# Tiles a quarter of a unit sooner, another order in units 0 and 1, and unread fp32 products in three waits of TensorE

## What is computed

```
for t in range(S):                       # 768 steps; B=4, H=8, D=48
    S_re, S_im = ar*S_re - ai*S_im + kv, ar*S_im + ai*S_re     # kv = k[t] outer v[t]
    y[t] = q[t] @ S_re                   # ar, ai: a_re, a_im scaled to magnitude <= 0.999
x = y as (3072, 384)
h = x @ w_in                             # (384, 2048)
g = where(h >= 1, h, where(h <= -1, 0, (h + 1)**2 / 4));   x = g @ w_out     # first layer
P = exp(x @ w_gate - max); eight times: rows normalised, columns normalised  # gate
out = sum over e of P[:, e] * (relu(x @ w1[e]) @ w2[e])                      # second layer
```

## Time and profile before

| | |
|---|---|
| median of 3 runs | 2300.43 us |
| lowest, highest | 2298.07, 2301.52 us |
| the profiled execution | 2298.59 us, its span 2296.8 us |
| mean granted TensorE clock | 0.994 of full |
| busy share of the span | PE 97%, DVE 75%, ACT 44%, POOL 20% |

### The profile page before, as it was taken

One profiled execution on the slowest core, in us unless ns is written; L12 is line 12 of the kernel. 1 busy time (PEld: TensorE's weight loads), 2 busy tenths in 40 slices (PEclk: granted clock), 3 DMA queues, 4 the chain that ended last, 5 costly groups with the idle time before them and its releaser, 6 DMA issues.

```text
span 2296.8 us, 37984 instructions
## 1 busy us (share of the span) xinstructions
PE 2226.7 (97%) x13699; PEld 2075.5 (90%) x13699; DVE 1733.0 (75%) x3049; ACT 1006.9 (44%) x1702; POOL 465.5 (20%) x310
## 2 busy tenths in 40 slices
PE   3899999999999899999999999999999999999999
PEld 3799999999999789999998899999998999999998
DVE  7898888888855867767778777777778777777775
ACT  3566666566555423343334333343333433344332
POOL 0000000000000422322323222332232222232222
PEclk9899999999999999999999999999999999999999
DMA  3311111111103031111111231011110211111111
GB/s 109 94 52 53 52 50 50 50 50 50 43 29 138 28 111 37 47 55 55 55 39 44 83 111 54 29 55 55 55 55 28 83 56 56 43 40 55 55 55 28
DMA packets 70725, 131.33 MB, mean 57 GB/s; under 512 B 5512, under 2 KB 36488, under 8 KB 70536
## 3 DMA queue, kind: packets, MB, share of 16 engines
q1 hardware_dynamic: 70536, 129.14, 17.4%
HBM read 114.96 MB, written 14.16 MB: 56 GB/s over the span
## 4 chain that ended last, share of the span: by engine, by line
PE 90%; DVE 8%; issue 1%; ACT 1%; DMA 0%; SPq 0%; DVEq 0%; ACTq 0%
PE bank L1547 16%; PE bank L1548 15%; PE bank L1549 15%; PE bank L1730 11%; PE bank L1732 11%; PE bank L1731 11%; PE bank L1527 2%; PE bank L1528 2%; PE bank L1518 1%; PE bank L1534 1%; PE bank L1493 1%; DVE tmp L947 1%; PE bank L1477 1%; DVE u_s L1334 0%; PE bank L1488 0%
## 5 line engine op out<-in xcount | busy, mean ns | idle before, releaser
L606 POOL TENSOR_TENSOR h_l<-u_s,h_h 128x512 fp32r<-128x512 f32 x192 | 245.0, 1298 | 1618.8 <-ACT h_h L854 1618.8
L1730 PE MATMUL bank<-w_h,h_h 128*128 128x384 f32 x1536 | 515.9, 336 | 11.1 <-DVE acc L1360 6.8
L1732 PE MATMUL bank<-w_h,h_l 128*128 128x384 f32 x1536 | 514.1, 335 | 0.0
L1731 PE MATMUL bank<-w_l,h_h 128*128 128x384 f32 x1536 | 514.0, 335 | 0.0
L1548 PE MATMUL bank<-x_l,w_h 128*128 128x512 f32 x1056 | 414.2, 392 | 0.0
L1547 PE MATMUL bank<-x_h,w_h 128*128 128x512 f32 x1056 | 414.0, 392 | 0.0
L1549 PE MATMUL bank<-x_h,w_l 128*128 128x512 f32 x1056 | 413.2, 391 | 0.0
L1360 DVE SCALAR_TENSOR_TENSOR acc<-bank,prob,acc 128x384 f32<-128x384 f32 x352 | 214.6, 612 | 174.3 <-PE bank L1732 171.5
L1730 PEld LDWEIGHTS bank<-w_h,h_h 128*128 128x128 f32 x1536 | 288.7, 188 | 16.8 <-DVE acc L1360 9.6
L1731 PEld LDWEIGHTS bank<-w_l,h_h 128*128 128x128 f32 x1536 | 288.8, 188 | 2.0
L1732 PEld LDWEIGHTS bank<-w_h,h_l 128*128 128x128 f32 x1536 | 288.7, 188 | 0.0
(11 more groups left out here) (188 smaller groups left out, 3976.1 us busy)
## 6 DMA issues: line engine op xcount, KB each, us to landing
stage<-w_ SPq DMA_DIRECT2D x48, 768.0 KB, 6.6
w_raw<-w_ SPq DMA_DIRECT2D x96, 384.0 KB, 3.6
qb<-q_in_ SPq DMA_DIRECT2D x24, 192.0 KB
kb<-k_in_ SPq DMA_DIRECT2D x24, 192.0 KB
vb<-v_in_ SPq DMA_DIRECT2D x24, 192.0 KB
x_hi<-x2h_s SPq DMA_DIRECT2D x36, 128.0 KB, 1.8
x_lo<-x2l_s SPq DMA_DIRECT2D x36, 128.0 KB, 1.8
x_h<-x_hi SPq DMA_DIRECT2D x3, 1536.0 KB, 10.5
```

The source lines that it names most:

```text
L606: pool.tensor_tensor(tiles_of(h_l, name), group_sum(name), tiles_of(h_h, name).bitcast(F32), ALU.subtract).then_inc(hl_done, 1)
L1730: pe.matmul(dst, h_h[:, f, t_], w2h[:, fw], start=n == 0, stop=False)
L1731: pe.matmul(dst, h_h[:, f, t_], w2l[:, fw], start=False, stop=False)
L1732: mm = pe.matmul(dst, h_l[:, f, t_], w2h[:, fw], start=False, stop=n == 3)
```

## The change

Four things change.

1. The tile of slot 0 is 4(u-2), so every unit works on tiles one further on and the tail after unit 23 has one tile fewer. In unit 2, `mm_in(0)` stands ahead of `p_by_tokens(2)`. `x2_hi` and `x2_lo` move up within even units, and the table `FIRST_LO` is spread otherwise.
2. In unit 0 DVE's `masked(0)` stands ahead of `scale(2)`; in unit 1 `masked(1)`, `state_add(1)` and `x_lo(1)` stand between parts of `blocks` and `scan`. ACT's `p_sq(2)` goes behind its last `first_lo`.
3. TensorE's `first_lo(0, 2)` moves from the end of unit 0 to a place behind `r_by_tokens(1)`, and the counters that tiles 0 wait for change with it.
4. TensorE gets `busy`: 14 products of 128x128 by 128x128 in fp32 once three steps of the first `scan` are done, 8 ahead of `r_by_tokens(0)`, 8 ahead of `y_sum(0)`. They write bank 7, and nobody reads them.

```diff
 # ScalarE
@@ def unit(u)
-                t = 4 * (u - 2) - 1
+                t = 4 * (u - 2)
@@ after tile_sq(t + 1)
+                if even and u >= 4:
+                    x2_hi(u // 2 - 2)
                 if even:
                     p_root(u + 1)
...
-                if even and u >= 4:
-                    x2_hi(u // 2 - 2)
                 tile_hi(t + 2)
...
                 y_out(u)
-                if not even and more:
+                if not even and more and u > 1:
                     p_sq(u + 1)
                 x_hi(u)
                 if u == 1:
                     first_lo(4, BY_PE)
+                    p_sq(2)
 # VectorE
@@ def first_unit()
                 p_sum(1)
+                masked(0)
                 scale(2)
-                masked(0)
                 p_inv(1)
@@ def second_unit()
                 by_q(1)
-                blocks(1, 1, 2)
                 k_by_r(1)
                 by_k(1)
-                blocks(1, 2, NI)
+                blocks(1, 1, 5)
                 masked(1)
+                blocks(1, 5, NI)
                 scan_init(1)
-                scan(1, 0, 4)
+                scan(1, 0, 2)
                 state_add(1)
+                scan(1, 2, 3)
+                x_lo(1)
+                scan(1, 3, 4)
                 final(2)
-                x_lo(1)
@@
-            FIRST_LO = {2: ((), (6, 7), (7, 8), (8, 10)), 3: ((10, 11), (11, 12), (12, 13), (13, 14)),
-                        4: ((14, 15), (15, 16), (), ())}
+            FIRST_LO = {2: ((6, 7), (7, 8), (), (8, 11)), 3: ((11, 12), (12, 13), (13, 14), (14, 15)),
+                        4: ((15, 16), (), (), ())}
@@ def unit(u)
-                t = 4 * (u - 2) - 1
+                t = 4 * (u - 2)
...
 # TensorE
+            def busy(n):
+
+                for _ in range(n):
+                    pe.matmul(bank[7][:, 0:128], ident[:], ones[:], start=True, stop=True)
@@ def mm_in(t), mm_out(t)
-                    pe.wait_ge(piece_l, PIECES.index((0, m)) + 1)
+                    pe.wait_ge(piece_l, PIECES.index((0, m)) + 1 if m else BY_PE - 1)
...
-                    pe.wait_ge(piece_l, PIECES.index((1, m)) + 1)
+                    pe.wait_ge(piece_l, PIECES.index((1, m)) + 1 if m else BY_PE)
@@ for u in range(UNITS)
-                t = 4 * (u - 2) - 1
+                t = 4 * (u - 2)
...
+                if u == 0:
+
+                    pe.wait_ge(scan_step, 2 + 3 * 3)
+                    busy(14)
+                if u == 2:
+
+                    mm_in(0)
                 p_by_tokens(u)
-                tile_in(t)
+                if u != 2:
+                    tile_in(t)
+                if u == 0:
+                    busy(8)
                 r_by_tokens(u)
+                if u == 1:
+                    first_lo(0, 2)
...
+                if u == 0:
+                    busy(8)
                 y_sum(u)
                 state_sum(u)
                 tile_in(t + 3)
                 x_by_channels(u)
-                if u < 2:
-                    first_lo(4 * u, 4 * u + 2)
+                if u == 1:
+                    first_lo(4, BY_PE)
...
-            for m in range(-1, TILES):
+            for m in range(TILES):
```

More of the change, by code:

```diff
@@ L1188, in unit @@
                 masked(u)
+                if even and u >= 4:
+                    x2_lo(u // 2 - 2)
                 tile_max(t + 1)
@@ L1201, in unit @@
                 tile_max(t + 2)
-                if even and u >= 4:
-                    x2_lo(u // 2 - 2)
                 if scans:
@@ L1295, in _ @@
                 unit(u)
-            g_max((GROUPS - 1) * TILES - 2)
-            for m in range(-1, TILES):
+            g_max((GROUPS - 1) * TILES - 1)
+            for m in range(TILES):
                 t = (GROUPS - 1) * TILES + m
```

## The result

The changed kernel takes **2303.42 us** (median of 19 runs, 2301.62 to 2305.63) against 2299.99 (19 runs, 2297.80 to 2301.52) before: ratio 1.0018, 95% interval 1.0012 to 1.0025. The profiled span is 2301.1 us for 2296.8, 4.3 us longer. The forecast was 2304.3 us, and the time lies in its range of 2295 to 2309. But the sum came out right by luck: the start gained 1.9 us less than said and the steady units lost 1.5 us less than said, and each of these errors is larger than the forecast's own miss of 0.9 us.

What follows compares the result with a forecast made beforehand. TensorE's work was taken to bound the steady units. From a span of 2298.59 us, less 2.7 for the start, plus 6.6 for steady waits, came 2302.5; with 1.84 up to the median, 2304.3 us, range 2295 to 2309.

Steps and rivals of the forecast that it cites:

- the start: Units 0 to 4: gain of 4.0 us, or 1.6 with the half clock in unit 1; taken as 2.7.
- the steady units: Even units 6 to 20: eight added waits for x2_lo, 8 x 0.82 = 6.6 us of cost.
- The bound: In the steady units time is the sum of TensorE's work; gains come only where TensorE idles or runs at half clock.
- Unit 0: masked(0) first: y_sum(0) starts at about 42.6 for 46.35; at full clock state_sum(0) ends at 47.6 for 55.8.
- The unread products: Unit 0: the fourteen cost between 0 and 1.5 us, each eight at most about 1; all taken as 0.
- Unit 1: by_q(1) at 54.0 for 60.02; first_lo(0, 2) takes 3.3 to 6 us; r_by_tokens(2) starts 4.0 (1.4) us sooner.
- Rival (a): Half clock at the start, between 47.6 and 54.8 and in y_sum(2): gain taken as 0.5, 2306.5 us, slower; chance 0.27.
- The rule that was weighed there: Unit 1: transposes don't bring the full clock, so it would fall, gain 1.6 or less; the profile row said 4.0.
- Units 2 to 4: masked(4) ends 2.3 us sooner (or 0.3 later); y_sum(4) at 157.1 (159.5) for 156.77, with 4.3 us more TensorE work done.
- The steady wait: Even units 6 to 20: TensorE idles about 0.8 us for VectorE's x2_lo ahead of the nought product.
- this doesn't heal: Steady units: VectorE has no gap to make up the x2_lo wait, so each of eight costs its whole 0.82 us.
- The tail: After the last unit, one tile fewer: slack of the loads falls from 8.5 to 4.2 us, cost 0.

## Why the prediction came out as it did

- **The bound** was read right. What moved the time is in the first 175 us and in the one new wait, but for 0.5 us by which the new order of TensorE's list is shorter from unit 5 to 23 (498.60 us without the wait for 499.14 before); the prediction had no term for that. The waits between 745 and 2300 us are the same in both traces.
- **Unit 0** was right: `y_sum(0)` at 43.38 (42.6 said) and at full pace, `state_sum(0)` over at 48.5 (47.6 said).
- **The unread products** were put at 0. The 14 took 6.0 us, all at half pace, and `p_by_tokens(0)` started at 32.04 for 30.40, past the prediction's upper bound of 1.5 by 0.1; of this 0.7 reached `r_by_tokens(0)`. With and without them the times can't be told apart, so the 0 holds for the sum.
- **Unit 1**: `r_by_tokens(1)` at 54.66 (by_q at 54.0 said, 54.52 measured), `q_and_k(1)` at 60.75 (58.1, or 60.7 with the half clock), `r_by_tokens(2)` at 84.00 (81.2, or 83.8). It was the slow end each time. Rival (a)'s sign came too: the first product of `first_lo(0, 2)` lasted 1.92 us for 1.02, with the clock down from 52 us on. The rule that was weighed there (the Trainium skill, page "TensorE: Matmul & The Clock Gate", Part 4, that transposes don't count as TensorE being busy) isn't settled by this: TensorE did not only have transposes and no products, it stood idle for 2.33 us ahead of them and for 2.58 behind.
- **Units 2 to 4: the step that failed.** `nought` was to start some 2 us before `y_sum` at 157.1 to 159.5; `y_sum(4)` came at 160.27. The step priced `mm_out` at its full-clock 2.12 us and left out that TensorE stands idle ahead of it. The idle time is 2.16 us, and it took the clock down. That is 1.6 us of the 1.9 that the gain of the start fell short of 2.7; the kernel with `x2_lo` ahead in unit 4 alone, and the one with products in that wait, both give it back. The other 0.3 is within what alike traces differ by. (Redone from its own terms, the prediction's `y_sum(4)` is at 157.2 or 159.8 for the 157.1 or 159.5 written, and its gain 3.9 or 1.3 us for 4.0 or 1.6; its 2.7 lies between either way.) Rival (a) had a start gain of 0.5 through a second half-clock stretch, the right size; but it put the stretch in `y_sum(2)`, where it did not come.
- **The steady wait** was the right mechanism at the right place, put down to `x2_lo` in every even unit from 6 to 20. The local delay is right as well: in unit 14 the nought product starts 1.02 us behind the product ahead of it, and 0.21 in the kernel without the wait, 0.81 more for 0.82 predicted (the 0.74 in the brackets is the idle part). What was off is "this doesn't heal": 0.70 of the 0.81 stays in the period. VectorE did not catch up, since all eight waits are 0.73 or 0.74 us; the steps between TensorE's products in units 14 and 15 add up to 0.14 us less than without the wait, and why stays open. With the 0.07 us by which the list is shorter, the period grew by 0.63, and the eight cost 5.1 us for 6.6.
- **The tail** gave nothing back, as said: the kernel with `first_lo(0, 2)` ahead of `r_by_tokens(1)`, 3.0 us ahead of the changed one at `r_by_tokens(23)`, is still 3.0 ahead where the wait near 805 us ends (804.1 for 807.1).
- So the sum -2.7 + 6.6 = 3.9 met the 4.3 us of the traces as -0.8 + 5.1, the 5.1 being 5.6 for the waits less 0.5 for the shorter list. That the two errors nearly cancelled is luck. (The shares of its chances add up to 0.34 slower and 0.55 same, for 0.33 and 0.56 written.)
- What the prediction did not look for: on the kernel before, `masked(0)` ahead of `scale(2)` alone is worth 4 us, and the tile shift alone costs 7 to 8. The nearly unchanged time is a loss and a gain of some us laid over each other.

## What to carry to other kernels

When a step that a busy engine waits for is moved, look at what stands directly ahead of it on the producing engine: a swap of two neighbours (1.0 us ahead of 1.3 us, the second with 1.6 us to spare) turned a loss into a gain here. Filling an engine's waits to hold its clock pays only where that engine is next waited for; ask who waits for the work that the clock speeds up before asking how to get the clock. And measure the parts of a change apart, since a change that measures as nothing can be a good part and a bad one.

## What the hardware showed that was not expected

- **A granted clock of 1.00 at the start of the records does not mean full pace.** In the changed kernel the stretch from 28 to 29 us and that from 32 to 33:

```profile
28.00:29.00 1.00, 1.00 (x7) 1.00 0.00 0
32.00:33.00 1.00, 1.00 (x11) 1.00 0.00 0
```

  Both say 1.00, but 7 instructions ran in the first and 11 in the second, all back to back, and the fp32 products of 128x128 (two instructions each in the records) took 0.43 us each, 14 in 6.0 us, where a score product of that shape took 0.21. They are the same products as the eight that follow at 32.70 and take 1.95 us. So the pace has to be read off the instructions there; the column does not show it.

- **The same list of instructions, another clock.** The kernel with `first_lo(0, 2)` ahead of `r_by_tokens(1)`, and the one with `x2_lo` ahead of `masked` too, are alike up to unit 4. In the stretch from 52 us, the first and then the second:

```profile
52.00:54.00 2.00, 2.00 (x6) 0.50 1.08 306
```

```profile
52.00:54.00 2.00, 2.00 (x9) 1.00 1.03 301
```

  The Trainium skill, page "TensorE: Matmul & The Clock Gate", Part 1, says that the chip's look at TensorE's activity runs free of the program, so that the same gap can fall well or badly. The two rows fit that. `r_by_tokens(4)` starts at 138.76 in the first and 137.39 in the second: a single trace can so be over 1 us off in the start, which is the size of most terms here.

- **Which waits were followed by a fall.** Eight waits of 0.74 us in the changed kernel left the clock at 1.00, and so did one of 0.90 to 0.98 in unit 4 in five kernels. The wait of 2.16 us in unit 4 was followed by a fall in this kernel's trace and in each of the others that had one of 2.1 to 2.3 us there (the kernels with `first_lo(0, 2)` moved, without products, with `masked(0)` put back, and with the shift alone). In between it is open: in the second layer every one of the 14 traces has a wait of 1.75 to 1.78 us between 1256 and 1273 us, ahead of the same product, and a fall follows it in five of them and not in the other nine. The changed kernel, and then the one with `first_lo(0, 2)` ahead of `r_by_tokens` (busy TensorE, PEclk, DMA share, GB/s):

```profile
1255.00:1275.00 20.00, 18.23 (x103) 1.00 0.00 1
1255.00:1275.00 20.00, 18.24 (x95) 0.91 0.00 1
```

  No edit of this document touches that place. Behind `r_by_tokens(23)` the eleven traces with the changed kernel's tiles took between 1622.4 and 1625.1 us, so a gain of 1 to 3 us at `r_by_tokens(23)` need not show in full in a median of 6 to 11 runs.
